# The last stage in pairs of tiles: first layer by seven block products, outputs delayed and cut in halves

## The reference

```python
def _moe2_ref(x, w_in, w_out, g_ln):          # x 2304x512, w_in 512x1024, w_out 1024x512
    h = x @ w_in
    h_max = np.max(h, axis=-1, keepdims=True)
    e = np.exp(h - h_max)
    sm = e / (np.sum(e, axis=-1, keepdims=True) + 1e-09)
    solu = h * sm
    mu = np.mean(solu, axis=-1, keepdims=True)
    var = np.mean((solu - mu) ** 2, axis=-1, keepdims=True)
    ln = (solu - mu) / np.sqrt(var + 1e-06) * g_ln
    return (ln @ w_out).astype(np.float32)
```

## Time and profile before

| | us |
|---|---|
| median of 3 runs (lowest, highest) | 1205.48 (1204.16, 1205.86) |
| the profiled execution's own time | 1204.52 |
| span of the profiled execution | 1202.6 |
| PE busy (share of the span) | 1180.2 (98%) |
| PEld busy | 1052.3 (88%) |
| DVE busy | 619.9 (52%) |
| ACT busy | 396.9 (33%) |
| POOL busy | 297.9 (25%) |
| mean granted TensorE clock | 0.999 of 2.4 GHz |

### The profile page before, as it was taken

One profiled execution on the slowest core, in us unless ns is written; L12 is line 12 of the kernel. 1 busy time (PEld: TensorE's weight loads), 2 busy tenths in 40 slices (PEclk: granted clock), 3 DMA queues, 4 the chain that ended last, 5 costly groups with the idle time before them and its releaser, 6 DMA issues.

```text
span 1202.6 us, 17044 instructions
## 1 busy us (share of the span) xinstructions
PE 1180.2 (98%) x6248; PEld 1052.3 (88%) x6248; DVE 619.9 (52%) x1125; ACT 396.9 (33%) x884; POOL 297.9 (25%) x275
## 2 busy tenths in 40 slices
PE   7999999999999999999999999999999989999997
PEld 7999999889988998998899899889989878888885
DVE  7878887644244534343533334443434566555562
ACT  6777787232223211113311112321111422222321
POOL 5667784242434200014300004400000300100000
PEclk9999999999999999999999999999999999999999
DMA  7777773775563313162505071505061200000000
GB/s 173 182 193 183 194 175 114 289 262 196 193 235 116 121 59 125 30 225 68 187 1 184 1 253 53 201 1 184 1 209 45 71 1 18 26 17 26 17 27 26
DMA packets 98730, 140.84 MB, mean 117 GB/s; under 512 B 40816, under 2 KB 69488, under 8 KB 98544
## 3 DMA queue, kind: packets, MB, share of 16 engines
q1 hardware_dynamic: 98672, 140.06, 37.0%
HBM read 105.16 MB, written 26.03 MB: 109 GB/s over the span
## 4 chain that ended last, share of the span: by engine, by line
PE 91%; ACT 3%; issue 3%; DVE 3%; DMA 0%; POOL 0%; POOLq 0%; ACTq 0%; DVEq 0%
PE s L1500 29%; PE outp L1368 25%; PE s L1368 22%; PE ring L1368 11%; PE ring L1379 3%; ACT ptr_h L828 1%; PE ring L1613 1%; DVE ptr_l L1080 1%; ACT pr L823 1%; PE outp L1579 1%; DVE probs_n L1232 0%; DVE w_l L1185 0%; DMA k_raw<-in_k 0%; DVE h_max L1312 0%; ACT w1s_h L843 0%
## 5 line engine op out<-in xcount | busy, mean ns | idle before, releaser
L1500 PE MATMUL s<-xr,w1s_h 128*128 128x384 f32 x1344 | 374.2, 337 | 0.3 <-DVE u L1288 0.3
L1500 PEld LDWEIGHTS s<-xr,w1s_h 128*128 128x128 f32 x1344 | 245.6, 188 | 8.0 <-DVE u L1288 0.7
L1500 PE MATMUL s<-xr,w1s_l 128*128 128x384 f32 x672 | 225.8, 336 | 0.0
L978 ACT ACTIVATE hid_h<-u 128x384 fp32r<-128x384 f32 x96 | 50.5, 526 | 382.2 <-DVE u L1288 260.4
L1500 PEld LDWEIGHTS s<-xr,w1s_l 128*128 128x128 f32 x672 | 126.3, 188 | 7.0
L1368 PE MATMUL s<-k_h,qb 128*128 128x288 f32 (+8 forms) x320 | 75.7, 325 | 7.0 <-DVE qb L1160 5.6
L823 ACT ACTIVATE pr<-s,neg_max 128x576 f32<-128x576 f32 (+2 forms) x144 | 75.0, 525 | 21.0 <-DVE neg_max L1073 17.7
L704 POOL TENSOR_TENSOR sums<-stage 128x256 f32<-128x256 f32 x16 | 11.8, 735 | 265.8 <-DMA stage<-in_moe_w 264.5
L1368 PE MATMUL ring<-w_h,hid_h 128*128 128x512 f32 x192 | 76.7, 399 | 0.0
L1368 PE MATMUL outp<-w_h,hid_h 128*128 128x512 f32 x192 | 76.4, 398 | 0.0
L1368 PE MATMUL s<-w_h,hid_h 128*128 128x512 f32 x192 | 75.8, 395 | 0.0
(11 more groups left out here) (151 smaller groups left out, 2454.5 us busy)
## 6 DMA issues: line engine op xcount, KB each, us to landing
xr<-x_stash SPq DMA_DIRECT2D x77, 768.0 KB, 6.0
stage<-in_moe_w SPq DMA_DIRECT2D x64, 256.0 KB, 5.0
x_stash<-x_tmp SPq DMA_DIRECT2D x12, 768.0 KB, 4.4
qb<-q_hl SPq DMA_DIRECT2D x30, 288.0 KB, 5.4
x_stash<-xr SPq DMA_DIRECT2D x1, 5376.0 KB, 16.7
k_raw<-in_k SPq DMA_DIRECT2D x16, 288.0 KB, 3.2
q_over<-in_q SPq DMA_DIRECT2D x16, 288.0 KB, 3.7
r_sb<-r_scratch SPq DMA_DIRECT2D x32, 144.0 KB, 3.1
```

Source lines behind the costliest of these rows:

```text
L978: act.activation(hid[slot][0][:, :], source[:, :], ACT.Relu).then_inc(hid_high, 1)
L1500: last = pe.matmul(target, x, y, start=start and i == 0, stop=stop and i == 2, skip_group_check=True)
```

## The change

Only the last stage changes, and the preparation of `w_in` for it.

- The 18 tiles become nine pairs (`TP`). A pair's first layer is computed by the seven block products: each is two blocks by three passes, so 42 matmuls of 512 columns for a pair in place of 48. The moving operand is the prepared `w_in`, read in four pieces of 128 columns; the stationary one is a set of seven blocks of the activations (`yop`).
- `w_in` is prepared as the experts' first weights are: all seven blocks, with the sums on POOL.
- The activations are turned from the accumulator directly; ACT copies them out (`y_copy`), POOL makes the sums (`y_add`) and the low parts, ACT the high parts.
- The hidden rows are collected in SBUF (`h_a`, `h_b`): ACT copies one block, DVE makes the other three with additions. Maximum, exponentials and softmax product read them from SBUF. The product and the normalisation are made in place in `ex`, of which there are two.
- The outputs use two banks and come later: the output of tile 2p-3 runs in pair p in two halves, and so does that of tile 2p-2.
- The loops over tiles are written out.

More of the change, by code:

```diff
@@ L636, in _ @@
                 first_halves(e + 1)
[L637 to L650, removed]
+                second_halves(e + 1, SUPERS * (e + 1))
+            for i in range(TT):
+                sp.wait_ge(o_copied, i + 1)
+                sp.dma_start(out[i * P:(i + 1) * P, :], o_sb[i % 2][:, :]).then_inc(stored[i % 2], 16)
+            for s in range(2):
+                sp.wait_ge(stored[s], 16 * TP)
         @block.gpsimd
@@ L778, in _, with y_operands @@
                     w1_low_plain(e, v)
+                    if (e, v) == (EXPERTS, HALF_F - 1):
+                        y_add(0)
                     w1_low_sums(e, v)
[L780 to L809, removed]
+            for s in range(2):
+                pool.memset(rstd[s][:, 1:2], -0.5).then_inc(consts_step, 1)
+            pool.wait_ge(consts_step, 3)
+            def y_operands(p):
+                y_add(p)
+                y_low_rows(p)
+                y_low_sums(p)
+            y_operands(1)
+            for p in range(TP):
+                reciprocal_root(p, 0)
+                if p == 0:
+                    y_operands(2)
+                reciprocal_root(p, 1)
+                if 1 <= p < TP - 2:
+                    y_operands(p + 2)
         @block.scalar
@@ L1025, in _ @@
                         unit(e, sg, u)
[L1026 to L1040, removed]
@@ L1057, in _, with y_copy @@
-            tile(0, 0)
-            tile(1, 1)
-            with act.Fori(1, TT // 2 - 1) as half:
-                tile(2 * half, 0)
-                tile(2 * half + 1, 1)
-            tile(TT - 2, 0)
-            tile(TT - 1, 1)
-            ln_high_part(TT - 1, 1)
+            def y_copy(p):
+                act.wait_ge(y_turned, p + 1)
+                if p >= 2:
+                    act.wait_ge(y_low, 2 * (p - 1))
+                elif p == 1:
+                    act.wait_ge(first_y_low, 2)
+                act.activation(y_t[:, :], s01[:, :], ACT.Copy).then_inc(y_copied, 1)
@@ new lines, in copy_out @@
+            def copy_out(i):
+                if i >= 2:
+                    act.wait_ge(stored[i % 2], 16 * (i // 2))
+                act.wait_ge(o_done, i + 1)
+                act.activation(o_sb[i % 2][:, :], out_bank(i), ACT.Copy).then_inc(o_copied, 1)
+            w1_cast_plain(EXPERTS, HALF_F - 1, 0)
+            w1_cast_plain(EXPERTS, HALF_F - 1, 1)
+            w1_cast_sums(EXPERTS, HALF_F - 1)
+            y_copy(0)
+            y_cast_rows(0)
+            split2(EXPERTS, 4, gained=True)
@@ new lines, in wide_c22, with wide_c21, wide_c12 @@
+            def wide_c22(p):
+                dve.wait_ge(h_prod, made(p, "m5"))
+                dve.wait_ge(h_comb, combined(p, "u3"))
+                if p >= 1:
+                    dve.wait_ge(solu_done, 2 * p)
+                dve.tensor_tensor(h_b[:, D:F], wide_x(p), hu3[:, :], ALU.add).then_inc(h_comb, 1)
+            def wide_c21(p):
+                dve.wait_ge(h_prod, made(p, "m4"))
+                dve.tensor_tensor(h_a[:, D:F], wide_y(p), hm1[:, :], ALU.add).then_inc(h_comb, 1)
+            def wide_c12(p):
+                dve.wait_ge(h_prod, made(p, "m3"))
+                dve.tensor_tensor(h_b[:, 0:D], wide_x(p), hu2[:, :], ALU.add).then_inc(h_comb, 1)
@@ L1345, in tile @@
-            def tile(t, par):
-                maximum(t, par)
-                if not (isinstance(t, int) and t == TT - 1):
-                    y_low_part(t + 1)
-                if not (isinstance(t, int) and t < 1):
-                    ln_low_part(t - 1, 1 - par)
-                normalise(t, par)
-            tile(0, 0)
-            tile(1, 1)
-            with dve.Fori(1, TT // 2 - 1) as half:
-                tile(2 * half, 0)
-                tile(2 * half + 1, 1)
-            tile(TT - 2, 0)
@@ L1359, in _ @@
-            tile(TT - 1, 1)
-            ln_low_part(TT - 1, 1)
+            wide_c22(0)
+            wide_c21(0)
+            maximum(0)
+            wide_c12(0)
+            maximum(1)
+            product_part(0)
[11 more added lines that the diff above has]
+            variance(1)
@@ L1625, in tile @@
-            def tile(t, par):
-                hidden(t, par)
-                if not (isinstance(t, int) and t == TT - 1):
-                    turn_y(t + 1)
-                if not (isinstance(t, int) and t < 1):
-                    turn_ln(t - 1)
-                if not (isinstance(t, int) and t < 2):
-                    output(t - 2, par)
-            pe.wait_ge(w_in_ready, HALF_F)
-            tile(0, 0)
-            tile(1, 1)
-            pe.wait_ge(w2_ready, (EXPERTS + 1) * FC)
-            with pe.Fori(1, TT // 2 - 1) as half:
-                tile(2 * half, 0)
-                tile(2 * half + 1, 1)
```

418 lines of the change are left out of this document (257 added, 161 removed).

## The result

| | before | changed |
|---|---|---|
| median, us (lowest to highest, 4 runs each) | 1204.82 (1202.74 to 1205.86) | 1244.12 (1237.95 to 1246.03) |
| profiled execution: time, span, us | 1204.52, 1202.6 | 1237.95, 1236.2 |
| mean granted TensorE clock in it | 0.999 | 0.985 |

The changed kernel is slower: ratio 1.032, 95% interval 1.0278 to 1.0361. Forecast were 1231.5 us and a range to 1242; the direction was right, the size too small by 12.6 us, and the time lies 2 us above the range. The profiled run is the fastest of the four; the other three had a mean granted clock of 0.977 to 0.979 against its 0.985.

The account below looks back on a forecast made before the run. PE's issued work was taken to bound the last stage. 957.6 start + 218.6 PE work + 39.7 waits + 3.2 tail = 1219.1; with 1.5 port and 8.0 clock, span 1228.6, time 1231.5 us; range 1216 to 1242.

Parts of the forecast that it names:

- What is removed, 54 x 0.233 us: PE, last stage: six matmuls of 512 columns fewer a pair, 12.6 us in all.
- The rival of the slow operand: First-layer matmuls: moving operand in four pieces is slower; 0.05 us on each of 378 makes 19 us, 1250; chance 0.03.
- The wait in each pair, 3.4 us: PE before output(2p-3, 0): chain from m3 to ln_low_part takes 5.7 us against 2.3 of other work; six times, 20.4 us.
- Maximum from SBUF at 1.23: DVE's maximum, in the chain to each output: reading SBUF takes 1.23 us, as from PSUM; other bound 0.83.
- the 3.2 us of the lower end: DVE's maximum at 0.83 us would take 0.4 off each of eight waits, 3.2 us.
- Start and end of the stage: PE waits 5.2 and 2.8 us before outputs 0 and 1, 4.8 and 2.6 before 15 and 16, 0.5 at turn_ln(17).
- The small waits of the start: Stage start: 1.3 us before hidden(0, "m1") and 2.1 together in pairs 0 and 1; 3.4 us.
- The port, 1.5 us: Pair 1: POOL's SBUF work delays DVE's product_part(1), in the chain to output(0, 0); 0 to 1.9 us, taken as 1.5.
- All waits together: PE over the last stage: all waits sum to 39.7 us, for a span of 1219.1 before port and clock.
- The clock: five falls at 1.6 us, 8.0 us: PE after waits: five of eight waits of 3.3 us and more lower the clock, 1.6 us each, 8.0 us.
- The rival in which the clock falls each time: PE: the clock falls after all ten waits, 1239.5 us, slow matmuls seen in every pair; chance 0.23.
- The expected gain of 23 us: Last stage, if nothing waited: 12.6 us of matmuls and 10.6 us of waits and slow clock would go.

Follow-up runs that it names:

- the earlier turn: Changed kernel with turn_ln(2p-1) ahead of output(2p-2, 1) on PE, and that tile's high part earlier on ACT, low part earlier on DVE, p from 2: 1204.25 us.
- the filled waits: Changed kernel with idle matmuls, result unused, put on PE in all ten waits before an output: 1223.14 us, ratio 1.0141.
- the second profile: The changed kernel run and profiled once more, with no edit: 1241.32 us, ratio 1.0302.

## Why the prediction was wrong, step by step

- *What is removed, 54 x 0.233 us.* Right. The products are issued 0.233 apart (2.80/12), with the moving operand in four pieces, and the pair without waits came to 23.38 for 23.4 forecast. The rival of the slow operand falls. (Of the work before, the 98.6 us of output matmuls should read 98.8, 18 x 5.49.)
- *The wait in each pair, 3.4 us.* Right in place, releaser and size: idle 3.20, and from 26.87 less 23.38 it costs 3.49. The order on ACT was shown to cause 2.17 of the 3.20 us (1.03 left by that edit); the earlier turn, with the order on DVE, took the rest.
- *Maximum from SBUF at 1.23.* It took 1.22, so the 3.2 us of the lower end were not to be had. The Trainium skill's table (VectorE: DVE Perf Modes, "The perf-mode tier table") has the plain mode alone for it, and the 1.22 us from SBUF beside 1.23 from PSUM agree.
- *Start and end of the stage.* Idle 4.83 and 2.65 before outputs 0 and 1 (5.2 and 2.8 forecast), 4.61 and 2.43 before 15 and 16 (4.8 and 2.6); `turn_ln(17)` had no wait of its own. The small waits of the start were 2.8 for 3.4.
- *The port, 1.5 us.* It did not come: `product_part(1)` took 1.38 us in place of 1.28. The product had begun first, and POOL lost: its addition beside it (`y_s`, L792) took 1.59 us in place of 0.74. In pairs 2 to 7 DVE lost, as one `normalise` a pair took 1.39 us for 0.81 beside POOL's first addition, off PE's chain, as forecast.
- *All waits together.* Forecast span without the clock 1220.6, with the port; from the two profiles 1220.5 and 1220.0, or 1220.7 by the filled waits. That it fits so well is in part luck. The forecast has 39.7 us of waits and 1.5 for the port. Idle were 36.5, and the restart took 0.28 us behind a wait (3.02 less 2.74) in place of 0.1, which for ten waits makes 39.3 in all, an estimate. Where the other 1.9 us went was not looked for.
- *The clock: five falls at 1.6 us, 8.0 us.* This is the step that failed. It was eight falls and 15.5 us in one profile, ten falls and 19.3 us in the other. Three timed runs had spans of 1240.6 to 1244.2, by the same rest 20 to 24 us. The mechanism was the one forecast, two sizes were off. The number: from the one wait of 3.21 us I had taken five of eight; 11 of 12 waits of that length were followed by a fall, and so were waits of 2.43 and 2.64 us. And the price: rows 4 and 5 showed one short stretch of 3.4 us, and I took 1.6 for each; three of eight and four of ten lasted 6.8 us and cost up to 2.8 here. The rival in which the clock falls each time had the ten falls of the second profile and, at 1.6 each, still 3.3 to 8 us too little. With it failed a small term: I had put the median run 1.0 us above the profiled one, as before; it lies 6.2 above, at the lower mean clock.

The expected gain of 23 us was turned into waits that cost some 41 us (1220.7 less 1202.6 - 23.2), 15.2 of them set up by the order of two instructions on ACT, and the waits then took 15 to 24 us more through the clock.

## What to carry to other kernels

In an in-order queue look, for each wait of the bounding engine, at what stands ahead of its releaser: an instruction for the newest tile ahead of one for the oldest makes the old one as late as the new. Price a PE wait of 2 us or more that comes back every turn with the slow stretch behind it, once for the number of falls and once for their length, and look for slow stretches in the whole span before a difference is put down to the stage that was changed. And filling such a wait with idle matmuls tells in one run which part is the wait and which the clock.

## What the runs showed of the hardware

- The slow stretches of TensorE's clock before the last matmul lasted 3.4 or 6.8 us, nothing between, over all profiles. The long ones of the changed kernel began 0.9 to 2.4 us before PE went on (1092.8 for 1093.65, 1065.9 for 1066.91), the short ones at most 0.5 us before it, or up to 1.3 us after. Only what PE would have issued in them costs, with output matmuls 0.43 us apart in place of 0.23.
- A fall is a matter of more than the idle time: of equal waits of 1.82 us one of six was followed by one, of 2.51 us two of six, of 3.20 us 11 of 12. The Trainium skill (TensorE: Matmul & The Clock Gate, "🎯 Why this matters for your kernels") warns of idle gaps between bursts of matmuls as what lowers the clock in the middle of a kernel. The rows agree that such gaps lower it. The gap that the page still lets pass is longer than 1.8 and 2.5 us, and after one of six and two of six such waits the clock fell here: in that the measurement differs, and decides. What else decides was not tried.
- The same changed kernel ran at 1237.85 to 1246.03 us in eight runs, the kernel before within 1202.74 to 1207.00. Number and length of the stretches explain it for the two profiled runs; for the others there is the mean clock alone.
- A slow stretch of 3.4 us can also stand in attention, some 16 us into the span: in four of the ten profiles of the changed kernel and its variants, which are the same there. The last stage then began at 958.58 to 959.15, otherwise at 956.85 to 957.93.
